# Gated linear attention with two expert layers: a new order of the first weights' product and unit 0, and three of its joins as plain fp32 matmuls

## Chip, cores and metric

One Trainium2 chip, one core. The metric is the device time of one execution in microseconds. TensorE (PE) does the matmuls and transposes, VectorE (DVE), ScalarE (ACT) and GpSimd (POOL) the elementwise work, and SyncE (SP) issues all DMAs, in one order.

## The reference

```python
for t in range(S):                        # q, k, v, f_logit: (4, 8, 768, 48)
    state = f[:, :, t, :, None] * state + einsum('bhd,bhe->bhde', k[:, :, t], v[:, :, t])
    y[:, :, t] = einsum('bhd,bhde->bhe', q[:, :, t], state)
x = y as (3072, 384)                      # f = sigmoid(f_logit)
h = x @ w_in                              # (384, 2048)
g = h if h >= 1, 0 if h <= -1, else (h + 1)**2 / 4
x = g @ w_out                             # (2048, 384)
out = ((x @ w1) * (x @ w2)) @ w3 @ w_last # (384, 1024) twice, (1024, 1024), (1024, 384)
```

All inputs are fp32. Since nothing stands between w3 and w_last (`moe2_w_out`), the kernel multiplies these two first and uses the product, w_joined (1024 x 384), in the last layer.

## The kernel before

**Units.** The 3072 tokens are 8 units of 384. For each unit there is an attention part and the first expert layer (w_in, gate, w_out), whose result goes to DRAM ("middle"). A second part then reads it in 6 groups of 512 and does the rest. Attention is done by halving blocks: within leaves of 4 tokens on VectorE and GpSimd (steps `gates`, `score0`, `sum`, `lag`, `prefix`, `query4`, `values`, `leaf_lag`, `leaf_add`), then transposes of the gates' total, of k and of q (`tot`, `k`, `q`), four levels of block scores (`level`, each followed on VectorE by masks, `k_next` and `q_next`, which the next level needs), key rows (`krow`), state updates (`update`), output (`y`) and its transposes (`x`).

**Precision.** Most matmuls run in three parts (`in_parts`, L1079): each operand is split in a high part, rounded to fp32r by ScalarE, and a low part, the difference, by VectorE; high by high, high by low and low by high are summed. The attention, the transposes and the fillers are plain fp32 matmuls.

**Joining w3 and w_last.** Eight row tiles of w3 are turned (`turn(t)`, L1085: 8 transposes into two banks), split by ScalarE (`turned_high`, L682) and VectorE (`turned_low`, L920) into two buffers, and joined with w_last (`join(t, part)`, L1098: 8 k tiles in 4 parts of 2, 24 matmuls in all). ScalarE copies the result (`joined_copy`, L689) and SyncE stores it to DRAM (L473). w_last itself is split once by `last_high` (L676) and `last_low` (L914); its low part takes the place of the raw values. All of this lies in the memory that w_out, x and g take later. So w_out is loaded after the joined rows have been stored (L474 to L478), and unit 0's `split_x` (L635) waits for that too.

**Order.** Each engine runs through the same positions, 32 to a unit; position 0 is where unit 0's first layer begins (`turn_of_units`: `up(0)`, `up(1)`). At odd positions TensorE does an `up` (w_in, 9 matmuls), at even ones a `down` (w_out, 9 matmuls). Tables written out by hand say at which position each step of the attention stands: `K_AT`, `LEVEL_AT` and the like (L236 to L243) for units 1 to 7, `UNIT0_AT` and `FIRST_AT` (less 32) for unit 0 and `NEXT_AT` for the steps ahead of unit 1. `JOIN_AT` (less 32) places the turns and the join parts, `LAST_AT` w_last's split, `PIECE_AT` the splits of w_in and w_out in 14 pieces. Within a position TensorE does attention first, then turns and joins, then `up` or `down`. Each engine executes strictly in its own order, so what stands behind a waiting instruction waits too. Narrow attention steps take one of three banks in turn, wide ones (`level`, `krow`, `update`, `y`) two of them; a step waits until the bank's last reader is done (`wait_bank`).

**Fillers.** `keep_running(n)` (L1151) issues n matmuls of the identity by itself whose result nobody reads: 40 before turn 0, 12 before turn 1, 12 before join 0, 9 before level 1 and 20 before level 3 of unit 0, 93 in all.

In TensorE's order, ahead of the first layer, the kernel has: turns 0, 1; total; join 0 among the transposes of k and q; turn 2, half of join 1; levels 0 to 3 with the rest of join 1 and turn 3; join 2 around the key rows; update 0; most of join 3; y 0; all other joins and turns at a stretch; then y 1, x 0, update 1, y 2, x 1, x 2, mixed with unit 1's first transposes.

Of the kernel before, what the change touches and what calls it, by code (L numbers as in the profile page):

```python
# [38 lines left out]
JOIN_PARTS = 4  # L39
GPSIMD_PIECES = ()  # L40
HEAD_ROWS = 64
GROUP = 512
BEFORE_TURN, BEFORE_JOIN, BEFORE_LEVEL = {0: 40, 1: 12}, 12, (0, 9, 0, 20)
# [51 lines left out]
def first_part(nc, given):  # L95
# [17 lines left out]
    with ExitStack() as ctx:  # L113
# [40 lines left out]
        pieces = halves_in[0:KD] + pairs_out[0:KD] + halves_in[KD:] + pairs_out[KD:]  # L154

        def in_piece(half, kk):
            return 2 * KD * half + kk

        def out_piece(i):
            return KD + i // 2 + (KD if i // 2 >= KD else 0)  # L160
# [4 lines left out]
              for n, o in (("hi", "w_out_hi"), ("lo", "w_out_lo"))]  # L165
        w3s = place("w3_rows", [P, 4, F2], over="x_hi")
# [5 lines left out]
        for name, shape in (("w1", [P, KD, F2]), ("w2", [P, KD, F2]), ("w_joined", [P, T2, DM])):  # L172
# [69 lines left out]
        GATES_AT, SCORE0_AT, SUM_AT, LAG_STEPS_AT, PREFIX_AT, QUERY_AT = 15, 1, (17, 27), (21, 22), 20, 28  # L242
        VALUES_AT, LEAF_LAG_AT, LEAF_ADD_AT = 17, 30, (31, 31)  # L243
# [158 lines left out]
        def _(sp):  # L402
# [89 lines left out]
            sp.wait_ge(joined_out, 16 * T2)  # L492
# [82 lines left out]
        def _(act):  # L575
# [161 lines left out]
        def _(dve):  # L737
# [176 lines left out]
            def last_low():  # L914
                for t in range(0, T2, 2):
# [4 lines left out]
            def turned_low(t):  # L920
                for half in range(2):
# [45 lines left out]
        def _(pe):  # L967
# [117 lines left out]
            def turn(t):  # L1085
# [306 lines left out]
```

## Time and profile before

| | |
|---|---|
| median of 3 runs | 948.19 us (947.43 to 951.37) |
| profiled execution | 946.54 us, of it 944.6 span |
| TensorE busy | 924.0 us, 98% |
| weight loads busy | 860.0 us, 91% |
| VectorE, ScalarE, GpSimd busy | 526.3, 392.5, 148.6 us |
| mean granted TensorE clock | 0.99 |
| chain that ended last | TensorE 93%, VectorE 5% |
| moved by DMA | 57.67 MB |

Idle time of an engine counts only where it lies on the chain that sets the end. Matmuls are pipelined: the duration of one (334 ns for 384 columns) is longer than the distance from one start to the next, and it is the distance that sets the pace. The trace names tiles by their place in memory: the w3 rows are `w_rows`, the turned ones `w_turned_hi` and `w_turned_lo`, the identity `ident`. A granted clock of 1.0 is 2.4 GHz, of 0.5 it is 1.2 GHz.

### The profile page before, as it was taken

Reading aid. Unit: us, or ns where it says so; the run is one execution under the profiler, and the core shown is the slowest. Engines: PE = TensorE matmul, PEld = TensorE weight load, DVE = VectorE, ACT = ScalarE, POOL = GpSimd, SP = SyncE. Lnnn points to the kernel's source line nnn. Section 1 sums busy time; section 2 is a strip of 40 time slices with the busy share of each in tenths; the row PEclk is TensorE's granted clock in tenths of the full one; section 3 lists DMA queues with packets and bytes.
Section 4 is the critical chain, followed back from the end, with each engine's and each line's share of the span. In section 5 each row is a group of like instructions: output and inputs, shape, how many; then the busy total and the mean of one; then the engine's idle time right before and its main releaser. Section 6 shows DMA issues by size and latency. Waiting matters only on the chain.

```text
span 944.6 us, 24359 instructions
## 1 busy us (share of the span) xinstructions
PE 924.0 (98%) x10722; PEld 860.0 (91%) x10722; DVE 526.3 (56%) x956; ACT 392.5 (42%) x766; POOL 148.6 (16%) x151
## 2 busy tenths in 40 slices
PE   6999799999999999999999999999999999999998
PEld 6989799999999999999999999998888888888887
DVE  6766698767767767768768664463222122213122
ACT  1433555645544644644644544674222222222212
POOL 2414104305205115115125000000000000000000
PEclk9999799999999999999999999999999999999999
DMA  9931820260340430530520200602020202000000
GB/s 267 247 119 43 210 52 2 66 88 2 78 76 2 89 66 2 97 58 1 112 43 2 52 2 2 248 12 93 1 67 1 67 1 68 1 34 0 34 1 34
DMA packets 115834, 57.67 MB, mean 61 GB/s; under 512 B 92433, under 2 KB 111121, under 8 KB 115217
## 3 DMA queue, kind: packets, MB, share of 16 engines
q1 hardware_dynamic: 115728, 56.11, 24.9%
q8 instruction: 85, 1.39, 0.6%
q14 instruction: 21, 0.16, 0.1%
HBM read 45.09 MB, written 11.01 MB: 59 GB/s over the span
## 4 chain that ended last, share of the span: by engine, by line
PE 93%; DVE 5%; DMA 1%; ACT 1%; issue 1%; SPq 0%; DVEq 0%; ACTq 0%
PE bank L1081 16%; PE bank L1083 15%; PE bank L1082 15%; PE bank L1327 11%; PE bank L1326 11%; PE bank L1325 10%; PE bank L1019 4%; PE bank L1056 2%; PE bank L1030 1%; PE bank L1062 1%; PE bank L1043 1%; PE bank L993 1%; DMA first_q<-in_q_dram 1%; PE bank L988 1%; PE bank L998 1%; PE bank L1076 1%
## 5 line engine op out<-in xcount | busy, mean ns | idle before, releaser
L1295 DVE TENSOR_TENSOR product<-bank,a_copy 128x512 f32<-128x512 f32 x48 | 33.2, 692 | 221.1 <-PE bank L1327 221.1
L1081 PE MATMUL bank<-x_hi,w_in_hi 128*128 128x384 f32 x384 | 135.4, 353 | 0.5 <-DVE x_lo L900 0.5
L1081 PE MATMUL bank<-g_hi,w_out_hi 128*128 128x384 f32 x384 | 133.6, 348 | 0.3 <-DVE g_lo L911 0.3
L1083 PE MATMUL bank<-x_hi,w_in_lo 128*128 128x384 f32 x384 | 129.2, 337 | 0.0
L1082 PE MATMUL bank<-x_lo,w_in_hi 128*128 128x384 f32 x384 | 129.0, 336 | 0.0
L1083 PE MATMUL bank<-g_hi,w_out_lo 128*128 128x384 f32 x384 | 128.7, 335 | 0.0
L1082 PE MATMUL bank<-g_lo,w_out_hi 128*128 128x384 f32 x384 | 128.6, 335 | 0.0
L657 ACT ACTIVATE g_hi<-gated 128x384 fp32r<-128x384 f32 x128 | 67.2, 525 | 128.2 <-DVE gated L906 128.2
L1327 PE MATMUL bank<-y_hi,w_lo 128*128 128x512 f32 x288 | 112.8, 392 | 0.0
L1326 PE MATMUL bank<-y_lo,w_hi 128*128 128x512 f32 x288 | 112.7, 391 | 0.0
L1325 PE MATMUL bank<-y_hi,w_hi 128*128 128x512 f32 x288 | 112.0, 389 | 0.0
L1249 ACT ACTIVATE a_copy<-bank 128x512 f32<-128x512 f32 x48 | 28.7, 598 | 187.2 <-PE bank L1327 187.2
L906 DVE SCALAR_TENSOR_TENSOR gated<-bank,gated 128x384 f32<-128x384 f32 x128 | 70.9, 554 | 59.6 <-ACT gated L651 59.5
L648 ACT ACTIVATE gated<-bank 128x384 f32<-128x384 f32 x128 | 62.4, 488 | 98.9 <-PE bank L1083 98.9
L911 DVE TENSOR_TENSOR g_lo<-gated,g_hi 128x384 fp32r<-128x384 f32 x128 | 71.6, 560 | 21.9 <-ACT g_hi L657 21.9
L1081 PEld LDWEIGHTS bank<-x_hi,w_in_hi 128*128 128x128 f32 x384 | 72.5, 189 | 2.8 <-DVE w_out_lo L392 0.6
L1081 PEld LDWEIGHTS bank<-g_hi,w_out_hi 128*128 128x128 f32 x384 | 72.0, 188 | 2.7 <-DVE g_lo L911 0.9
L534 POOL TENSOR_TENSOR y_leaf<-q_leaf,k_leaf 96x384 f32<-96x384 f32 x28 | 32.8, 1197 | 264.6 <-PE bank L998 234.9
L1082 PEld LDWEIGHTS bank<-x_lo,w_in_hi 128*128 128x128 f32 x384 | 72.6, 189 | 0.0
L1083 PEld LDWEIGHTS bank<-x_hi,w_in_lo 128*128 128x128 f32 x384 | 72.4, 188 | 0.0
L1082 PEld LDWEIGHTS bank<-g_lo,w_out_hi 128*128 128x128 f32 x384 | 72.2, 188 | 0.0
L1083 PEld LDWEIGHTS bank<-g_hi,w_out_lo 128*128 128x128 f32 x384 | 72.1, 188 | 0.0
(115 smaller groups left out, 1729.7 us busy)
## 6 DMA issues: line engine op xcount, KB each, us to landing
v_leaf<-in_v_dram SPq DMA_DIRECT2D x8, 576.0 KB, 6.5
v_rows<-in_v_dram SPq DMA_DIRECT2D x64, 72.0 KB, 2.7
middle<-middle_out SPq DMA_DIRECT2D x8, 576.0 KB, 3.3
w_rows<-in_moe_w_dram SPq DMA_DIRECT2D x8, 512.0 KB, 10.1
f_leaf<-in_f_logit_dram SPq DMA_DIRECT2D x28, 144.0 KB, 3.8
k_leaf<-in_k_dram SPq DMA_DIRECT2D x28, 144.0 KB, 4.6
q_leaf<-in_q_dram SPq DMA_DIRECT2D x28, 144.0 KB, 4.4
out_dram<-out_rows SPq DMA_DIRECT2D x5, 768.0 KB, 4.0
```

The lines of the kernel that those rows point to most:

```text
L648: nc.scalar.activation(gt[:, i % RING], h_bank[i % 2][:, 0:UNIT], ACT.Relu, bias=0.5, scale=0.5)\
L657: nc.scalar.activation(g[0][:, i % RING], gt[:, i % RING], ACT.Copy).then_inc(sems["g_hi"], 1)
L906: nc.vector.scalar_tensor_tensor(gt[:, i % RING], h_bank[i % 2][:, 0:UNIT], 1.0, gt[:, i % RING], ALU.max, ALU.min).then_inc(sems["gated"], 1)
L911: nc.vector.tensor_tensor(g[1][:, i % RING], gt[:, i % RING], g[0][:, i % RING].bitcast(F32), ALU.subtract)\
L1019: last = nc.tensor.matmul(wide[to:to + keys, pair // 2, o:o + HALF], kw[head_rows(ab), pair, at_:at_ + keys], later_half, start=True, stop ...
L1081: nc.tensor.matmul(o, w[0], b[0], start=first, stop=False)
L1082: nc.tensor.matmul(o, w[0], b[1], start=False, stop=False)
L1083: return nc.tensor.matmul(o, w[1], b[0], start=False, stop=last_)
L1295: nc.vector.tensor_tensor(pf[:, f % RING], b_bank[f % 2][:, 0:GROUP], af[:, f % 2], ALU.mult)\
L1325: nc.tensor.matmul(o, w[0], b[0], start=first, stop=False)
L1326: nc.tensor.matmul(o, w[0], b[1], start=False, stop=False)
L1327: return nc.tensor.matmul(o, w[1], b[0], start=False, stop=last_)
```

## The change

- Joins 0 to 2 (`PLAIN = 3`) are plain fp32 matmuls of the turned w3 rows by raw w_last, one per k tile. Their turned rows are copied by ScalarE unrounded and have no low part. The next turn waits for ScalarE's copy there, no longer for VectorE's low part.
- w_last comes in four loads, each with its own semaphore, behind the first w3 rows; part n of join 0 waits for load n. w_last's split stands behind update 0, its low part waits for join 2, and part n of join 3 waits for its share of it.
- The tables are new. TensorE's order ahead of the first layer becomes: turns 0, 1; total; join 0 among the transposes of k and q; level 0; turn 2, half of join 1, leaf 0, level 1, rest of join 1, leaf 1, level 2; turn 3, level 3, leaf 2; join 2 around the key rows, update 0; y 0, turn 4, join 3 with x 0, y 1, update 1, x 1, y 2 between its parts; turn 5, join 4 with x 2 before its last part; turn 6, join 5, turn 7, joins 6 and 7; then k 0, total, q 0, k 1, q 1, q 2 of unit 1. On VectorE the prefix of unit 0 comes behind the sums, w_last's low split ahead of y 0's add, and unit 1's lag steps on either side of turn 7's low part.
- Fillers: 20 before turn 0, 16 before turn 1, 3 before level 0, 8 before level 1, 8 before level 3, 55 in all.
- Of w_out's four loads only the last waits for the stored joined rows. Unit 0's `split_x` waits for turn 6, and its first `high` for the first four stored joined rows.
- All six pieces of w_in are split ahead of w_out's eight.

```diff
+PLAIN = 3
...
-BEFORE_TURN, BEFORE_JOIN, BEFORE_LEVEL = {0: 40, 1: 12}, 12, (0, 9, 0, 20)
+BEFORE_TURN, BEFORE_JOIN, BEFORE_LEVEL = {0: 20, 1: 16}, 0, (3, 8, 0, 8)
...
-        pieces = halves_in[0:KD] + pairs_out[0:KD] + halves_in[KD:] + pairs_out[KD:]
+        pieces = halves_in + pairs_out
...
+        wt_plain = place("w3_turned_plain", [P, 2, T2, P], over="w3_turned_hi")
...
-        K_AT, TOTAL_AT, Q_AT = (-7, -4, -1, 1), -3, (-2, -1, 0, 0)
-        Q_NEXT_AT, K_NEXT_AT = (3, 7, 9, 15), (4, 7, 11, 13)
-        LEVEL_AT = (3, 7, 9, 12)
-        LEAF_AT, KROW_AT, UPDATE_AT, Y_AT, X_AT = (8, 9, 15), (15, 22), (16, 25), (18, 23, 28), (23, 27, 29)
+        K_AT, TOTAL_AT, Q_AT = (-7, -1, 2, 2), -2, (-2, -1, -1, 0)
+        Q_NEXT_AT, K_NEXT_AT = (6, 7, 8, 14), (5, 7, 11, 12)
+        LEVEL_AT = (4, 7, 9, 12)
+        LEAF_AT, KROW_AT, UPDATE_AT, Y_AT, X_AT = (7, 11, 13), (15, 20), (16, 25), (18, 23, 28), (20, 28, 29)
...
-        LAST_AT, MASKS_AT = -43, -60
-        JOIN_AT = (-49, -47, -37, -37, -26, -25, -24, -18, -17, -13, -9, -9, 4, 7, 9, 12, 12, 13, 13, 14, 15, 15, 15, 15, 16, 16, 16, 16, 17, 18, 18, 18, 18, 18, 19, 19, 19, 20, 21, 21)
+        LAST_AT, MASKS_AT = 10, -60
+        JOIN_AT = (-47, -46, -44, -37, -34, -29, -24, -24, -16, -13, -13, -5, 1, 4, 10, 11, 12, 12, 13, 15, 16, 16, 17, 17, 17, 18, 18, 18, 18, 18, 19, 19, 20, 20, 21, 22, 22, 22, 22, 22)
...
-        PIECE_AT = (-8, 6, 18, 28, 29, 30, 31, 33, 33, 36, 39, 43, 43, 44)
-        FIRST_AT = (-56, -55, -58, -57, -57, -61, -60, -58, -44, -60, -40, -29, -24)
-        UNIT0_AT = (23, 28, 29, -33, -30, -27, -24, -41, -29, -29, -27, -25, -14, -14, -8, -1, -14, -11, -6, 6, 9, 13, 24, 15, 22, 26, -16, -17, -10, -13, -6, -9, 7, -3, 30)
-        NEXT_AT = (4, 28, 12, 19, 20, 15, 17, 14, 23, 27, 26, 32, 37)
+        PIECE_AT = (-7, 3, 4, 17, 20, 26, 28, 29, 31, 37, 37, 38, 41, 43)
+        FIRST_AT = (-55, -39, -60, -58, -55, -62, -62, -54, -50, -58, -41, -34, -27)
+        UNIT0_AT = (13, 15, 18, -36, -33, -27, -27, -45, -35, -35, -32, -27, -25, -14, -8, -4, -15, -9, -2, 3, 6, 10, 14, 12, 13, 16, -16, -20, -14, -12, -8, -10, 6, -4, 19)
+        NEXT_AT = (18, 27, -30, 18, 25, 18, 21, -17, 22, 30, 27, 34, 38)
...
+            def load_w_last(part):
+                src = w_last[F2 * part // JOIN_PARTS:F2 * (part + 1) // JOIN_PARTS, :].rearrange("(t p) n -> p t n", p=P)
+                sp.dma_start(wl_raw[:, T2 * part // JOIN_PARTS:T2 * (part + 1) // JOIN_PARTS], src).then_inc(w_last_in[part], 16)
+
             load_first()
-            sp.dma_start(wl_raw[:], w_last.rearrange("(t p) n -> p t n", p=P)).then_inc(w_last_in, 16)
-            for t in range(4):
+            load_w3(0)
+            for part in range(JOIN_PARTS):
+                load_w_last(part)
+            for t in range(1, 4):
                 load_w3(t)
...
-                sp.dma_start(w_joined[:, t], joined_rows(t)).then_inc(joined_out, 16)
-            sp.wait_ge(joined_out, 16 * T2)
+                sp.dma_start(w_joined[:, t], joined_rows(t)).then_inc(first_joined_out if t < T2 // 2 else joined_out, 16)
             for n in range(WO_LOADS):
+                if n == WO_LOADS - 1:
+                    sp.wait_ge(first_joined_out, 16 * (T2 // 2))
+                    sp.wait_ge(joined_out, 16 * (T2 // 2))
...
-                    act.wait_ge(joined_out, 16 * T2)
+                    act.wait_ge(turned, 2 * (T2 - 1))
...
+                elif i == 0:
+                    act.wait_ge(first_joined_out, 16 * (T2 // 2))
...
             def last_low():
+                dve.wait_ge(joined, PLAIN)
...
-                for half in range(2):
+                for half in range(2) if t >= PLAIN else ():
...
                 for kk in range(T2 * part // JOIN_PARTS, T2 * (part + 1) // JOIN_PARTS):
-                    last = in_parts(y_acc[t % 2][:, 0:DM], [w[:, t % 2, kk] for w in wt], [w[:, kk] for w in wl],
-                                    kk == 0, kk == T2 - 1)
+                    if t < PLAIN:
+                        last = nc.tensor.matmul(y_acc[t % 2][:, 0:DM], wt_plain[:, t % 2, kk], wl_raw[:, kk],
+                                                start=kk == 0, stop=kk == T2 - 1)
+                    else:
+                        last = in_parts(y_acc[t % 2][:, 0:DM], [w[:, t % 2, kk] for w in wt], [w[:, kk] for w in wl],
+                                        kk == 0, kk == T2 - 1)
```

## Rows read from the trace of the kernel before

**Rows 1.** Busy time by stage: length, PE, PEld, DVE, ACT, POOL; then clock, DMA share, GB/s.

```profile
0.00:92.45 92.45, 81.43 (x1086) 78.08 (x1089) 65.29 (x85) 29.13 (x49) 29.31 (x44) 0.98 0.64 171
92.45:108.19 15.74, 10.13 (x210) 8.20 (x210) 8.40 (x24) 6.01 (x13) 5.02 (x6) 0.64 0.79 236
108.19:944.60 836.41, 832.49 (x9431) 773.75 (x9431) 452.65 (x848) 357.32 (x706) 114.22 (x102) 1.00 0.20 46
```

**Rows 2.** Timeline of TensorE, 0 to 110: start, us, line, operands, count, [idle before].

```profile
2.85 11.66 PE L1154 MATMUL bank<-ident 128*128 128x128 f32 x80 [2.85 <-POOL ident L508]
...
17.41 2.84 PE L1154 MATMUL bank<-ident 128*128 128x128 f32 x24
24.03 1.16 PE L1094 MATMUL bank<-ident,w_rows 128*128 128x128 f32 x8 [3.77 <-DVE w_turned_lo L923]
25.03 0.76 PE L981 MATMUL bank<-ident,f_leaf 96*112 96x96 f32 x4
...
39.94 1.60 PE L1019 MATMUL bank<-q_cols,k_cols 48*64 48x32 f32 x96
...
44.74 1.60 PE L1019 MATMUL bank<-q_cols,k_cols 48*64 48x32 f32 x96 [0.99 <-DVE scores L860]
...
57.24 1.01 PE L1019 MATMUL bank<-q_cols,k_cols 48*32 48x32 f32 x96 [0.56 <-DVE q_cols L819]
...
60.41 1.11 PE L1030 MATMUL bank<-ident,k_cols 48*64 48x48 f32 x48 [0.88 <-DVE scores L860]
...
70.74 0.33 PE L1056 MATMUL bank<-v_rows,scores 64*64 64x48 f32 x8
```

**Rows 3.** Timeline of TensorE: 21 matmuls of a join, and the first layer's first.

```profile
79.44 0.33 PE L1081 MATMUL bank<-w_last_hi,w_turned_hi 128*128 128x384 f32 x1
...
82.91 0.34 PE L1083 MATMUL bank<-w_last_hi,w_turned_lo 128*128 128x384 f32 x1
...
108.19 0.66 PE L1081 MATMUL bank<-x_hi,w_in_hi 128*128 128x384 f32 x1 [0.28 <-DVE x_lo L900]
```

**Rows 4.** Timeline of VectorE, 0 to 130.

```profile
20.74 2.54 DVE L776 TENSOR_REDUCE leaf_scores<-score_lags 96x48 f32<-96x2304 f32 x1
...
28.33 4.18 DVE L918 TENSOR_TENSOR w_last_lo<-w_last_raw,w_last_hi 128x768 fp32r<-128x768 f32 x4
...
68.20 2.44 DVE L879 SCALAR_TENSOR_TENSOR state<-state,total_chunk,bank 112x48 f32<-112x48 f32 x12
```

**Rows 5.** Busy time by stage, 25.4 to 28.4: the granted clock is third from the end.

```profile
25.40:28.40 3.00, 3.00 (x16) 3.00 (x15) 3.00 (x4) 3.00 (x5) 3.00 (x3) 0.50 0.90 225
```

**Rows 6.** Timeline of GpSimd: one blocked multiply, then unit 1's prefix, queries and values.

```profile
26.75 4.95 POOL L554 TENSOR_TENSOR y_leaf<-v_leaf,leaf_scores 96x384 f32<-96x384 f32 x1
...
83.11 3.61 POOL L541 TENSOR_TENSOR f_leaf<-f_leaf 96x384 f32<-96x384 f32 x3 [13.72 <-DVE k_leaf L787]
86.89 4.76 POOL L548 TENSOR_TENSOR q_leaf<-q_leaf,f_leaf 96x384 f32<-96x384 f32 x4 [0.17 <-POOL f_leaf L541]
...
94.28 3.18 POOL L554 TENSOR_TENSOR y_leaf<-v_leaf,leaf_scores 96x384 f32<-96x384 f32 x4
```

**Rows 7.** The w_out load: its issue, the queue's wait, us to landing, ScalarE's first split.

```profile
94.87 2.26 SPq L478 DMA_DIRECT2D w_out_raw<-in_moe_w_out_dram  x4
...
SPq L478 <- DMA w_joined<-joined_rows: 1.5, 1, 1.5
...
w_out_raw<-in_moe_w_out_dram SPq DMA_DIRECT2D x1, 768.0 KB, 4.6
...
104.03 0.83 ACT L664 ACTIVATE w_out_hi<-w_out_raw 128x768 fp32r<-128x768 f32 x1
```

**Rows 8.** TensorE's longest wait from 120 to 660, and unit 2's levels 0 and 1.

```profile
PE bank L1019 <- DVE k_cols L838: 0.3, 1, 0.3
...
186.99 1.60 PE L1019 MATMUL bank<-q_cols,k_cols 48*64 48x32 f32 x96
...
194.97 1.60 PE L1019 MATMUL bank<-q_cols,k_cols 48*64 48x32 f32 x96
```

More of the change, by code:

```diff
@@ L153, in first_part @@
                      for t in range(0, T1, 2)]
-        pieces = halves_in[0:KD] + pairs_out[0:KD] + halves_in[KD:] + pairs_out[KD:]
+        pieces = halves_in + pairs_out
         def in_piece(half, kk):
-            return 2 * KD * half + kk
+            return KD * half + kk
         def out_piece(i):
-            return KD + i // 2 + (KD if i // 2 >= KD else 0)
+            return 2 * KD + i // 2
         wl = [place(f"w_last_{n}", [P, T2, DM], F32R, over=o) for n, o in (("hi", "w_out_hi"), ("lo", "w_out_lo"))]
@@ L201, in first_part @@
         w_landed = [ctx.enter_context(nc.semaphore(f"w_landed{i}")) for i in range(KD + WO_LOADS)]
-        w_last_in, wl_hi, wl_lo, turned, turned_hi, turned_lo, joined, joined_ev, y_first_in = (
+        wl_hi, wl_lo, turned, turned_hi, turned_lo, joined, joined_ev, y_first_in = (
             ctx.enter_context(nc.semaphore(n)) for n in (
-                "w_last_in", "w_last_hi", "w_last_lo", "turned", "turned_hi", "turned_lo", "joined", "joined_evacuated",
+                "w_last_hi", "w_last_lo", "turned", "turned_hi", "turned_lo", "joined", "joined_evacuated",
                 "y_first_in"))
-        joined_out = ctx.enter_context(nc.semaphore("joined_out"))
+        first_joined_out, joined_out = (ctx.enter_context(nc.semaphore(n)) for n in ("first_joined_out", "joined_out"))
+        w_last_in = [ctx.enter_context(nc.semaphore(f"w_last_in{i}")) for i in range(JOIN_PARTS)]
         given["first"].update(second)
@@ L234, in first_part @@
         ROUND = 2 * T1
[L236 to L239 removed]
+        K_AT, TOTAL_AT, Q_AT = (-7, -1, 2, 2), -2, (-2, -1, -1, 0)
+        Q_NEXT_AT, K_NEXT_AT = (6, 7, 8, 14), (5, 7, 11, 12)
+        LEVEL_AT = (4, 7, 9, 12)
+        LEAF_AT, KROW_AT, UPDATE_AT, Y_AT, X_AT = (7, 11, 13), (15, 20), (16, 25), (18, 23, 28), (20, 28, 29)
         SPLIT = 30
[L242 to L246 removed]
+        GATES_AT, SCORE0_AT, SUM_AT, LAG_STEPS_AT, PREFIX_AT, QUERY_AT = 16, 14, (17, 27), (21, 22), 24, 30
+        VALUES_AT, LEAF_LAG_AT, LEAF_ADD_AT = 17, 31, (31, 31)
+        LAST_AT, MASKS_AT = 10, -60
+        JOIN_AT = (-47, -46, -44, -37, -34, -29, -24, -24, -16, -13, -13, -5, 1, 4, 10, 11, 12, 12, 13, 15, 16, 16, 17, 17, 17, 18, 18, 18, 18, 18, 19, 19, 20, 20, 21, 22, 22, 22, 22, 22)
         MASK_JOIN_AT = -62
[L248 to L251 removed]
+        PIECE_AT = (-7, 3, 4, 17, 20, 26, 28, 29, 31, 37, 37, 38, 41, 43)
+        FIRST_AT = (-55, -39, -60, -58, -55, -62, -62, -54, -50, -58, -41, -34, -27)
+        UNIT0_AT = (13, 15, 18, -36, -33, -27, -27, -45, -35, -35, -32, -27, -25, -14, -8, -4, -15, -9, -2, 3, 6, 10, 14, 12, 13, 16, -16, -20, -14, -12, -8, -10, 6, -4, 19)
+        NEXT_AT = (18, 27, -30, 18, 25, 18, 21, -17, 22, 30, 27, 34, 38)
         steps = [(at, ("x", n)) for n, at in enumerate(X_AT)]
@@ L346, in turned_rows @@
         def turned_rows(part, t, half):
-            return wt[part][:, t % 2, half * T2 // 2:(half + 1) * T2 // 2].rearrange("p k n -> p (k n)")
+            to = wt_plain if t < PLAIN else wt[part]
+            return to[:, t % 2, half * T2 // 2:(half + 1) * T2 // 2].rearrange("p k n -> p (k n)")
         def padded_pair(t, pair, j):
@@ L491, in _ @@
                 sp.dma_start(second[name][2][:], src.rearrange("(k p) n -> p k n", p=P)).then_inc(later_in[n], 16)
-            sp.wait_ge(joined_out, 16 * T2)
+            sp.wait_ge(joined_out, 16 * (T2 // 2))
             sp.dma_start(second["w_joined"][2][:], w_joined).then_inc(later_in[2], 16)
@@ L676, in last_high @@
             def last_high():
-                act.wait_ge(w_last_in, 16)
                 for t in range(0, T2, 2):
+                    act.wait_ge(w_last_in[t * JOIN_PARTS // T2], 16)
                     hi, raw_ = (w[:, t:t + 2, :].rearrange(flat) for w in (wl[0], wl_raw))
@@ L1089, in turn @@
                 for half in range(2):
-                    if t:
-                        pe.wait_ge(turned_lo, 2 * (t - 1) + half + 1)
+                    if t > PLAIN:
+                        pe.wait_ge(turned_lo, 2 * (t - 1 - PLAIN) + half + 1)
+                    elif t:
+                        pe.wait_ge(turned_hi, 2 * (t - 1) + half + 1)
                     for j in range(T2 // 2):
@@ L1102, in join @@
                         keep_running(BEFORE_JOIN)
+                    pe.wait_ge(w_last_in[part], 16)
+                if t == PLAIN:
                     pe.wait_ge(wl_lo, T2 // 2 * (part + 1) // JOIN_PARTS)
                 if part == 0:
-                    pe.wait_ge(turned_lo, 2 * t + 2)
+                    if t < PLAIN:
+                        pe.wait_ge(turned_hi, 2 * t + 2)
+                    else:
+                        pe.wait_ge(turned_lo, 2 * (t - PLAIN) + 2)
                     if t >= 2:
@@ L1108, in join @@
                 for kk in range(T2 * part // JOIN_PARTS, T2 * (part + 1) // JOIN_PARTS):
-                    last = in_parts(y_acc[t % 2][:, 0:DM], [w[:, t % 2, kk] for w in wt], [w[:, kk] for w in wl],
-                                    kk == 0, kk == T2 - 1)
+                    if t < PLAIN:
+                        last = nc.tensor.matmul(y_acc[t % 2][:, 0:DM], wt_plain[:, t % 2, kk], wl_raw[:, kk],
+                                                start=kk == 0, stop=kk == T2 - 1)
+                    else:
+                        last = in_parts(y_acc[t % 2][:, 0:DM], [w[:, t % 2, kk] for w in wt], [w[:, kk] for w in wl],
+                                        kk == 0, kk == T2 - 1)
                 if part == JOIN_PARTS - 1:
@@ L1116, in up @@
                     wait(pe, "gated", u, i - 1)
+                elif u == 0:
+                    pe.wait_ge(turned_lo, 2 * (T2 - 1 - PLAIN) + i + 1)
                 if u == 0 and i % (T1 // 2) == 0:
```

## Prediction

> **Where the time goes now.** I read the stages first [rows 1]. From 108.19 us, where the first matmul of the first layer starts, to the end TensorE is busy for 832.5 of 836.4 us at full clock, and the change adds or removes no matmul there. The page's first part says the same of the whole: TensorE 98% busy, VectorE 56%, ScalarE 42%, GpSimd 16%. What it can win lies in the 108.2 us ahead: in the first 92.45 us w3 and w_last are joined beside unit 0's attention, in the next 15.7 us unit 0's tail runs alone, TensorE 10.1 us busy with a mean granted clock of 0.64.
>
> Next TensorE in order of time [rows 2]. The first two rows shown are fillers (`keep_running`); a filler is two instructions of some 0.11 us each (24 in 2.84 us). The kernel has 93 fillers, 80 of their 186 instructions in 11.66 us at the start. The reader is to see the marks of the attention chain: total transposed at 25.03, level 0 at 39.94, level 1 at 44.74, level 3 at 57.24, the keys' rows at 60.41, first y at 70.74. Three of them idle behind VectorE, so VectorE's steps between levels set the pace. Joins fill the holes: 21 matmuls in 3.47 us plus one step, 0.1735 us each [rows 3], 4.17 us a join (24 matmuls), 1.04 a part.
>
> **Plain joins.** Joins 0 to 2 lose the split: per k tile one fp32 matmul for three fp32r ones. Nothing here shows a plain one of 384 columns. A filler is plain, of 128 columns, and two instructions of 0.11; three times the columns give at most 0.33 an instruction, 0.66 a tile. The low bound is two instructions at the fp32r pace, 0.35; the high one four, 0.69. I take 0.66, nearest in kind: 1.32 a part, 5.28 a join, 1.11 more than now, +3.3 us for three (-4.2 to +4.0). It frees VectorE of three turned lows (3.8 us, estimated from 0.65 a half) and moves 4.18 us of w_last lows [rows 4] from 28.33 to behind join 2.
>
> **Start to level 0.** The first w3 rows and w_last are ahead of need in either order: join 0 now stands behind the total's transpose, and that waits for the prefix. VectorE does score, prefix and two sums, ending at 23.28 [rows 4]; the new order puts prefix last, so the total moves from 25.03 to 23.3. From there (durations without a row of their own are read off TensorE's timeline of the first 110 us, as start to start): transposes 0.6, four parts 5.3, eight groups of k and q at 0.4, three fillers 0.7: 9.8, level 0 at 33.1. But TensorE now has idled since turn 1 (over by about 19, when w3's second rows land). Before, an idle of 3.77 us [rows 2] was followed by 3.0 us at granted 0.50, that is 1.2 GHz [rows 5]. I take half clock from 23.3 to about 28.5: 2.6 us lost (0 to 2.6; which of the two hangs on how long the new gap of 4.3 us is in truth). Level 0 at 35.7, 4.2 earlier. Unit 0's `query4` (1.9 in VectorE's timeline) follows to 25.1, and the leaves' lag and adds, held by GpSimd, end near 35: in time for level 0's masks at 37.3. Should GpSimd end at 35.7, as it does now, they end at 38.7; level 1 still starts when TensorE is free. The Trainium skill, "TensorE: Matmul & The Clock Gate", section "Why this matters for your kernels", asks for continuous matmuls, since idle gaps throw the clock back; it speaks against the 38 fewer fillers, and the trace agrees by that row. By a rule that an idle gap is free the sum would be 2.6 us lower.
>
> **Levels.** Level 0 takes 1.6; behind it stand turn 2 (0.95), two parts, a leaf (0.35), eight fillers (1.8): level 1 at 43.0. From level 0 to 1 was 4.8 with 3.2 of VectorE work in it; now that is hidden. Level 1 1.6, two parts and a leaf: level 2 at 47.6, where VectorE also arrives. Level 2 1.6 and 3.0 of VectorE: level 3 at 52.2. Its 1.0, a w_in low (1.2), turn 3's low (1.3), masks and keys 2.1: key rows at 56.8 (before 60.41). Then the state update waits for ScalarE, which splits two w_in pieces (1.05 each in its timeline) between the two key-row copies: update at 61.2, rest of join 2 to 64.6. VectorE finishes 12 state steps (2.44) [rows 4] at 65.35, which frees the banks: first y at 65.4, 5.3 ahead of 70.74. But by 70.74 the old kernel also had turn 4 and three parts done, 4.1 us.
>
> **Rest of the joins.** Left are three y (1.0 each), three x (0.45), an update 0.75, four turns at 0.95, five joins 20.8: 29.8 us. Two waits are new. w_last's lows (4.18) stand on VectorE ahead of y 0's add, and x 0 waits for it: 1.5 us. y 2 waits for the second 12 state steps: 1.1. The last join ends at 65.4 + 29.8 + 2.6 = 97.8, against 92.45, with the tail inside it.
>
> **From last join to first layer.** Two chains run side by side. (a) The w_out load no longer waits for all joined rows: it was issued at 94.87, 1.5 us of that a wait [rows 7]; now 0.9 us after the join. It lands after 4.6, at 103.3; ScalarE then splits two pieces (0.83 each) ahead of unit 1's total and q 0: 105.7, and q 1, q 2 need those banks. (b) Unit 1's lag products now stand on VectorE behind the turn lows and end about 95.2; GpSimd's prefix 3.6 and query 4.8 [rows 6] follow: q 0 at 103.6. Both end together: first layer at 106.7, 1.5 us before 108.19. Half clock follows the idle as before, 2.2 us then; I take 1 us more of it, 0.5 lost.
>
> **The other units.** Level 0 moves one place later and level 1 stays. They start 8.0 us apart, now 6.3: 1.6 of level, three expert steps of 1.56. VectorE's work in those 4.7 us, by its own timeline from 188.73 on, is masks 1.0, keys 1.2, queries 0.9 and two gate steps 1.0, together 4.1; margin 0.6, so zero. Were the margin gone, each tenth would cost 0.7 us over seven units (0 to +2). Keys and queries of pairs 2 and 3, total, lag and update steps move by a place or two the same way, TensorE's and GpSimd's order of them being kept but for q 1 and q 2 ahead of the turn; I cost them at nothing, since TensorE finds its next work ready throughout. TensorE's longest wait there now is 0.3 [rows 8].
>
> **Sum.** 944.6 - 1.5 + 0.5 = 943.6 of span; with the 1.9 outside it this execution would take 945.5. Its own time, 946.5, lies 1.6 below the median of the runs, 948.2; from the median the sum is 947.2. I give 946.4, between.
>
> **Rivals.** *The clock holds* (or turn 1 comes later than I think): no half clock at 23.3, 2.6 us, and full clock from 106.7, 1.6 us: together 4.2 below the forecast, 942. For: a late w3 row leaves a shorter gap. Against: the gap of 4.3 us is longer than the one that cost the clock. *GpSimd blocked*, the slower one: chain (b) is now last, with VectorE's sum, w_in low and lag beside it. One of GpSimd's multiplies took 4.95 us while VectorE worked without a break, against 0.8 usually (four in 3.18) [rows 6]; each such block is 4.1 more. One is +2.6 net; two of the seven put the first layer at 114.9 and the time at 946.4 + 8.2, 954.6. It decides once chain (b) is over 6.5 us late. Against: in the same work now (3.61 and 4.76) none was seen. The Trainium skill, "SBUF — State Buffer", section "Who interferes with whom", says one of the two engines blocks fully while the other holds the shared port; the 4.95 agrees. *It doesn't do what it says*: w3 first and w_last in four loads win nothing, since the prefix is last; that is in my forecast, and if a plain tile costs 0.35 the joins win 2 us more, still within noise: 944.5.
>
> **Chances.** A measurement of this kernel tells 0.5% from no change: 4.7 us. Forecast 0.58 (0.05 of it faster), the clock holds 0.22, GpSimd blocked 0.10, cheap plain joins 0.10. Faster 0.27, same 0.63, slower 0.10. The range reaches into the clock case, 941.0, and to one block, 951.0.
>
> **What would show it.** Plain records of about 0.33 us spacing, 48; a granted 0.5 around 23 to 28; total at 23.3, level 0 near 35.7, first y near 65; an idle ahead of x 0 ended by VectorE; last join near 98; first layer near 106.7 released by the q copies; then 836 us as before. Wrong if the first layer starts before 103 or after 111, or if that last stretch differs by over 2 us.

## The result and the profile after

The changed kernel takes 952.75 us in the median of 20 runs (946.76 to 956.0), the kernel before 947.14 on the same chips (20 runs): a ratio of 1.0057, 95% interval 1.0045 to 1.0068, so slower by 0.57%. That is past the 0.5% that the prediction calls no change, though the interval begins just below it, and the time lies outside its range of 941.0 to 951.0. The profiled execution took 952.83, of it 950.9 span; that span is 6.3 more than before. First the stages, cut at the same two events as in [rows 1]: end of the last join part, first matmul of the first layer.

```profile
0.00:101.30 101.30, 83.62 (x1170) 71.08 (x1171) 69.67 (x103) 33.19 (x56) 20.86 (x39) 0.93 0.58 156
101.30:110.76 9.46, 3.33 (x25) 3.00 (x23) 7.05 (x5) 5.06 (x9) 9.29 (x7) 0.76 0.84 288
110.76:950.90 840.14, 834.00 (x9433) 774.36 (x9431) 458.36 (x844) 353.93 (x702) 120.69 (x107) 1.00 0.21 47
```

The last join ends 8.85 us later than before, the tail behind it is 6.28 shorter, and from the first layer on it takes 3.73 more. The prediction had +5.35, -6.8 and +0.5. In the last stage 1.5 us of the 3.7 are busy time (834.0 against 832.5), the rest is idle time, 6.1 us in place of 3.9. The granted clock of the first stage fell from 0.98 to 0.93.

TensorE's timeline of the changed kernel, the marks of [rows 2] and the new waits:

```profile
23.06 0.89 PE L996 MATMUL bank<-ident,f_leaf 96*112 96x96 f32 x4 [4.51 <-DVE f_leaf L776]
...
34.71 1.60 PE L1034 MATMUL bank<-q_cols,k_cols 48*64 48x32 f32 x96 [0.24 <-ACT q_cols L610]
...
54.26 0.26 PE L1034 MATMUL bank<-q_cols,k_cols 48*32 48x32 f32 x5 [1.77 <-issue]
...
57.39 1.37 PE L1045 MATMUL bank<-ident,k_cols 48*64 48x48 f32 x48
...
66.14 0.33 PE L1071 MATMUL bank<-v_rows,scores 64*64 64x48 f32 x8 [0.59 <-DVE state L893]
...
71.50 0.52 PE L1091 MATMUL bank<-ident,y_rows 128*128 128x128 f32 x3 [2.11 <-DVE y_rows L901]
...
79.26 0.33 PE L1071 MATMUL bank<-v_rows,scores 64*64 64x48 f32 x8 [1.13 <-DVE state L893]
...
108.27 0.86 PE L1008 MATMUL bank<-ident,q_leaf 96*112 96x96 f32 x4 [5.65 <-POOL q_leaf L560]
...
110.76 0.67 PE L1096 MATMUL bank<-x_hi,w_in_hi 128*128 128x384 f32 x1
...
128.92 1.84 PE L1034 MATMUL bank<-q_cols,k_cols 48*64 48x32 f32 x96 [1.49 <-DVE q_cols L833]
...
143.08 1.01 PE L1034 MATMUL bank<-q_cols,k_cols 48*32 48x32 f32 x96 [0.59 <-DVE k_cols L852]
...
152.76 0.76 PE L1058 MATMUL bank<-v_rows,k_rows 64*48 64x48 f32 x48 [0.79 <-ACT k_rows L625]
```

The reader is to see five waits of 1.5 us and over, from the total on: ahead of the total, inside level 3 (an "issue": TensorE stood still and the profile shows nothing that it waited for; 91 of the level's 96 matmuls were done; I call this the instruction wait), ahead of x 0, ahead of unit 1's q 0, and ahead of its level 1. The next view is busy time by stretch of the same kernel, with the granted clock third from the end. Behind or in each of the five lies one at about half clock:

```profile
21.20:28.00 6.80, 4.94 (x11) 2.99 (x12) 5.99 (x6) 0.90 (x2) 4.95 (x3) 0.52 1.20 239
55.30:58.70 3.40, 3.40 (x53) 1.92 (x51) 1.25 (x3) 0.22 (x1) 0.00 (x0) 0.54 0.05 17
72.35:75.75 3.40, 3.40 (x65) 3.14 (x58) 1.08 (x4) 0.49 (x1) 0.00 (x0) 0.54 0.02 5
106.50:113.30 6.80, 5.03 (x25) 5.06 (x26) 4.84 (x4) 4.65 (x8) 6.80 (x5) 0.52 1.10 357
130.40:133.80 3.40, 3.40 (x28) 3.33 (x23) 3.40 (x7) 0.90 (x2) 0.00 (x0) 0.54 0.01 4
```

In three of them TensorE is busy throughout, so that up to half their length, 1.7 us each, is lost; the kernel before had its long stretch of half clock in the tail, where TensorE mostly had nothing to do ([rows 1], clock 0.64). The Trainium skill, "TensorE: Matmul & The Clock Gate", section "Why this matters for your kernels", warns of idle gaps, and the length that it gives for them is longer than any of these three; the waits of 1.8, 2.1 and 1.5 us here were followed by half clock as well, so for this kernel the measurement decides: shorter ones can count too.

Two waits have their cause on the other engines, in the timelines of VectorE (w_last's lows, then unit 0's round) and GpSimd (unit 1's prefix and queries):

```profile
65.95 5.07 DVE L933 TENSOR_TENSOR w_last_lo<-w_last_raw,w_last_hi 128x768 fp32r<-128x768 f32 x4
...
125.50 1.83 DVE L396 TENSOR_TENSOR w_out_lo<-w_out_raw,w_out_hi 128x768 fp32r<-128x768 f32 x2 [0.20 <-ACT w_out_hi L678]
...
127.72 0.95 DVE L833 TENSOR_TENSOR q_cols<-q_cols,total 112x768 f32<-112x768 f32 x1
```

```profile
63.86 4.61 POOL L546 TENSOR_TENSOR y_leaf<-q_leaf,k_leaf 96x384 f32<-96x384 f32 x4 [32.77 <-DVE q_cols L833]
...
98.38 3.59 POOL L553 TENSOR_TENSOR f_leaf<-f_leaf 96x384 f32<-96x384 f32 x3 [29.91 <-DVE k_leaf L801]
102.13 5.99 POOL L560 TENSOR_TENSOR q_leaf<-q_leaf,f_leaf 96x384 f32<-96x384 f32 x4 [0.17 <-POOL f_leaf L553]
```

The lows took 5.07 us in place of 4.18 [rows 4], and GpSimd's four multiplies, 63.86 to 68.47, lie beside their first half. The chain of work that ended last in the changed kernel (start, length, what) parts them:

```profile
66.04 3.03 DVE w_last_lo L933 x2
69.21 1.81 DVE w_last_lo L933 x2
```

Two beside GpSimd took 1.5 us each, two without it 0.9. `query4` took 5.99 in place of 4.76 [rows 6]. And level 1 of unit 1 waits for queries that stand on VectorE behind two w_out lows.

### The profile page after: what moved, and what is told of

Same layout as the page of the kernel before. It is cut to its first block, busy times and chain, and to the rows that moved or that the text cites. A ratio compares the mean times of both kernels' runs of the same rounds, so it can differ in the third digit from the quotient of the medians.

```text
span 950.9 us, 24157 instructions
## 1 busy us (share of the span) xinstructions
PE 920.9 (97%) x10622; PEld 848.4 (89%) x10622; DVE 535.1 (56%) x950; ACT 392.2 (41%) x766; POOL 150.8 (16%) x151
## 4 chain that ended last, share of the span: by engine, by line
PE 90%; DVE 5%; issue 1%; DMA 1%; POOL 1%; ACT 1%; SPq 0%; DVEq 0%; POOLq 0%
PE bank L1096 15%; PE bank L1098 14%; PE bank L1097 14%; PE bank L1355 10%; PE bank L1354 10%; PE bank L1353 10%; PE bank L1034 5%; PE bank L1132 2%; PE bank L1071 2%; PE bank L1045 1%; PE bank L1008 1%; PE bank L1077 1%; PE bank L1003 1%; PE bank L1058 1%; DMA first_q<-in_q_dram 1%
## 5 line engine op out<-in xcount | busy, mean ns | idle before, releaser
L925 DVE TENSOR_TENSOR g_lo<-gated,g_hi 128x384 fp32r<-128x384 f32 x128 | 75.9, 593 | 32.0 <-ACT g_hi L671 32.0
L546 POOL TENSOR_TENSOR y_leaf<-q_leaf,k_leaf 96x384 f32<-96x384 f32 x28 | 35.0, 1277 | 239.5 <-PE bank L1013 206.7
```

Of the source, the lines that this page charges most:

```text
L546: nc.gpsimd.tensor_tensor(yl[:, j], qj[:, j], kj[:, j], ALU.mult)\
L925: nc.vector.tensor_tensor(g[1][:, i % RING], gt[:, i % RING], g[0][:, i % RING].bitcast(F32), ALU.subtract)\
```

## The experiments

Each was timed against the kernel before on its own chip, where that took 946.6 to 946.7. "After" is the changed kernel, 952.75.

| run | what it is | median us | ratio (95%) |
|---|---|---|---|
| f1_fill | after, 48 more fillers | 946.62 | 0.9996 (0.9987 to 1.0005) |
| f2_pieces | after, last w_out splits later | 952.6 | 1.0057 (1.0042 to 1.0073) |
| f3_plain0 | after, no plain joins | 957.04 | 1.0105 (1.0092 to 1.0118) |
| f4_addfirst | after, w_last's split behind y 0's add | 953.45 | 1.006 (1.0046 to 1.0073) |
| g1_steady | f1, old tables for units 1 to 7 | 943.32 | 0.9963 (0.9951 to 0.9975) |
| g2_pieces | f1, last w_out splits later | 944.98 | 0.9986 (0.9978 to 0.9995) |
| g3_bfill | before, fillers at start and tail | 946.41 | 0.9989 (0.998 to 0.9999) |
| g4_all | g1, fewer fillers, two orders mended | 940.53 | 0.9945 (0.9929 to 0.9962) |
| h1_fillplain0 | f1, no plain joins | 959.04 | 1.013 (1.0115 to 1.0146) |
| h2_tailfill | before, fillers in the tail alone | 945.09 | 0.9983 (0.9973 to 0.9994) |
| h3_nofill | g4 without its added fillers | 947.45 | 1.0005 (0.9995 to 1.0015) |
| h4_lastfirst | f1, w_last loaded ahead of w3 | 952.22 | 1.0052 (1.0037 to 1.0066) |

**Is it the clock?** Fillers in three of the waits, and nothing else.

```diff
+BEFORE = {(0, "tot"): 18, (0, "x", 0): 8, (1, "q", 0): 22}
...
                     keep_running(BEFORE_LEVEL[n])
+                keep_running(BEFORE.get((u, *grp), 0))
```

> The changed kernel with fillers in three of its idle gaps, none longer than the gap: 18 ahead of unit 0's total (gap 4.5 us), 8 ahead of x 0 (2.1 us), 22 ahead of unit 1's q 0 (5.6 us). Theory clock (the gaps let the clock fall, and half clock after them is what costs): the granted clock rises from 0.987 to about 0.993, the half clock after 23, after 72 and after 106 is gone, and the time falls by 1.5 to 2 us for each of the three, 4 to 6 us in all, to about 947. Theory waits (the gaps themselves cost, the clock is a symptom): the fillers change the clock and not the time, 952 to 953. Theory plain price: no change either.

946.62, 6.1 less than the changed kernel (5.8 by the two ratios), with more for TensorE to do. Its timeline:

```profile
22.94 0.54 PE L998 MATMUL bank<-ident,f_leaf 96*112 96x96 f32 x4 [0.45 <-DVE f_leaf L777]
...
32.31 1.60 PE L1036 MATMUL bank<-q_cols,k_cols 48*64 48x32 f32 x96 [0.23 <-ACT q_cols L611]
...
49.12 1.01 PE L1036 MATMUL bank<-q_cols,k_cols 48*32 48x32 f32 x96 [0.38 <-DVE q_cols L834]
...
61.52 0.33 PE L1073 MATMUL bank<-v_rows,scores 64*64 64x48 f32 x8 [0.60 <-DVE state L894]
...
96.51 5.10 PE L1184 MATMUL bank<-ident 128*128 128x128 f32 x44
102.36 0.51 PE L1010 MATMUL bank<-ident,q_leaf 96*112 96x96 f32 x4 [0.75 <-POOL q_leaf L561]
...
104.16 0.42 PE L1098 MATMUL bank<-x_hi,w_in_hi 128*128 128x384 f32 x1
```

The total starts when it did (22.94), but level 0 is 2.4 us earlier, first y 4.6 and the first layer 6.6. Level 3 runs in one piece of 96: the instruction wait is gone too. So the fillers did more than their theory says. Of the 6.6 us, 2.4 come between the total and level 0, where nothing but the clock differs; 1.4 between the first y and the last join, and 0.6 behind it. The other 2.2 come between level 3 and the first y, where this run adds no filler: the instruction wait and the half clock behind it went together, and the run doesn't part them. Without these 2.2 the theory's places give 4.4. Its stretches, with the clock third from the end, show full clock from the total to the first layer; the wait of 1.49 us ahead of unit 1's level 1 has no filler, and half clock follows it:

```profile
22.90:104.16 81.26, 74.68 (x1164) 64.31 (x1164) 59.37 (x91) 32.76 (x59) 23.89 (x19) 1.00 0.52 146
122.80:129.60 6.80, 6.80 (x65) 6.74 (x58) 4.61 (x8) 2.03 (x4) 0.00 (x0) 0.50 0.23 49
```

**The wait in unit 0's round.** The last five w_out splits moved from positions 37 to 43 to 42 to 58, behind unit 1's queries, on the changed kernel and on f1.

```diff
-        PIECE_AT = (-7, 3, 4, 17, 20, 26, 28, 29, 31, 37, 37, 38, 41, 43)
+        PIECE_AT = (-7, 3, 4, 17, 20, 26, 28, 29, 31, 42, 46, 50, 54, 58)
```

> The changed kernel with the last five w_out splits placed shortly ahead of their use (positions 10, 14, 18, 22, 26 of unit 0 for 5, 5, 6, 9, 11). If the 3.7 us that came after the first layer's start are VectorE's burst of w_out lows ahead of unit 1's level 1 (idle 1.5 + 0.6 + 0.8 us and 3.4 us at half clock behind it), the stretch from the first layer to the end falls from 840.1 to about 836.4 and the time by 3.5 to 4 us, to 949. If they come from the new places of the levels and key rows in units 1 to 7, the stretch stays near 840.

952.6, nothing won: the wait of 1.49 is gone, but three of about 1 us stand later in the round (1.05 for k, 1.03 for the key rows, 1.08 ahead of an x), and the instruction wait in level 3 was 2.4 us in this run. A wait moved, not removed.

> The filled kernel with the last five w_out splits later (positions 10, 14, 18, 22, 26). In the run without fillers this took away the wait ahead of level 1 and put two of 1.0 us behind level 2 and the key rows. Here the clock is full when the first layer starts, so what these waits do to the clock shows: 839 us after the first layer's start and 944.5 if they do not lower it, 841 and 946.5 if they do.

944.98, 1.6 less than f1: the same waits of about 1 us, and behind them no half clock, so that from the first layer on it takes 838.5 us instead of f1's 841.1. On the changed kernel, too, that stage went from 840.1 to 839.2, but the first layer was 0.5 later.

**The plain joins.** The changed kernel, and then f1, with all joins split; `LAST_AT` as in the kernel before, since join 0 then needs both parts of w_last.

```diff
-PLAIN = 3
+PLAIN = 0
...
-        LAST_AT, MASKS_AT = 10, -60
+        LAST_AT, MASKS_AT = -43, -60
```

> The changed kernel with no plain joins: all eight in three parts, w_last split at its old place ahead of join 0. Theory plain price (0.66 us a tile, 1.1 us more for each join on TensorE, and w_last's lows in a worse place): 3 to 5 us faster, 948 to 950. Theory clock: join 0 waits for the split from 25 to about 30, level 0 comes near 40 again, so the last join ends no earlier; within 2 us of 952.7 either way.

957.04, 4.3 us slower instead of faster.

> The changed kernel with the fillers of the first experiment (18 ahead of unit 0's total, 8 ahead of x 0, 22 ahead of unit 1's q 0) and joins 0 to 2 in three parts again, w_last split ahead of join 0 as in the kernel before. With plain joins these fillers gave 946.6. Theory (the plain joins are worth something only because w_last's split and turn 0's low part then stand on VectorE ahead of turn 1 and join 0, so turn 1 waits some 9 us and everything behind it is late): about 950.5, 4 us more than with plain joins, as without the fillers (957.0 against 952.7). Rival (what the plain joins saved there was granted clock, which the fillers give back): 947 or less, as 3.3 us of TensorE work go away (1.1 a join).

959.04: 12.4 slower than f1, three times what the theory asked. TensorE's timeline of f3 (first row) and of h1 (the other fence):

```profile
26.21 1.94 PE L1111 MATMUL bank<-ident,w_rows 128*128 128x128 f32 x8 [9.03 <-DVE w_turned_lo L938]
```

```profile
26.14 1.94 PE L1113 MATMUL bank<-ident,w_rows 128*128 128x128 f32 x8 [7.88 <-DVE w_turned_lo L939]
...
33.10 0.50 PE L998 MATMUL bank<-ident,f_leaf 96*112 96x96 f32 x4
```

Turn 1 waits for turn 0's low part, which starts on VectorE at 25.4, behind all leaf steps up to `query4`; with plain joins turn 1 starts at about 17.4, with fillers and without. In h1 the 18 fillers then follow it (5.4 us here, partly at half clock, where they took 4.2 in f1 and filled a wait), and the total comes at 33.10 in place of 22.94. Behind that h1 also has two instruction waits, 2.42 us ahead of join 0 and 2.09 in level 2, though it has all of f1's fillers; how much of its 12.4 us they make wasn't parted. So a plain join does cost TensorE what the prediction said, and what it wins here is that VectorE's splits leave the start. The theory named the right wait; that fillers placed for one order become plain cost in the other it did not foresee. I read 4.3 us as what it costs to take the plain joins out of this order. It is no fair price of them by themselves: the tables were made for plain joins, and the kernel before, whose tables put turn 0's low part ahead of `query4`, has 3.77 us at the same place where f3 waits 9.03 [rows 2]. An order of split joins with new tables of its own was not run.

**Load order.** f1 with all of w_last ahead of w3's first rows.

```diff
-            load_w3(0)
             for part in range(JOIN_PARTS):
                 load_w_last(part)
-            for t in range(1, 4):
+            for t in range(4):
                 load_w3(t)
```

> The changed kernel with the fillers of the first experiment and w_last's four loads issued ahead of w3's first rows, otherwise the same; it stood at 946.6 with w3's rows first. Theory (turn 0 stands behind the first fillers and its rows land ahead of need only when first): turn 0 starts later by the time that 1.5 MB take, and as VectorE's first steps cover the total's wait, what is lost is hidden behind the fillers ahead of the total: 946.1 to 947.1. Rival (turn 0 and turn 1 and so the whole start shift by some 4 us): 950.

952.22: the rival is right. TensorE's timeline:

```profile
16.74 1.97 PE L1112 MATMUL bank<-ident,w_rows 128*128 128x128 f32 x8 [7.82 <-DMA w_rows<-in_moe_w_dram]
...
24.11 1.04 PE L1112 MATMUL bank<-ident,w_rows 128*128 128x128 f32 x8
...
29.00 0.49 PE L997 MATMUL bank<-ident,f_leaf 96*112 96x96 f32 x4
```

Turn 0 starts at 16.74 instead of 11.89, the fillers behind it run at half clock, and the total, ready on VectorE since about 23, starts 6.1 us later.

**w_last's lows behind y 0's add.** `LAST_AT` 12 for 10, on the changed kernel.

> The changed kernel with w_last's split behind y 0's add on VectorE and ScalarE instead of ahead of it. The idle of 2.1 us ahead of x 0 is gone, join 3's first part waits about 1 us more. Theory clock: the half clock after 72 goes with it, 1.0 + 1.7 us, so 2 to 3 us faster, 950. Theory waits: 1 us faster, 951.7.

953.45, unchanged within the scatter. The wait ahead of x 0 is gone, one of 1.4 us ahead of join 3 (for the same lows) has come, and the first layer starts 2.7 us earlier in the profile; but that execution (950.65) lies at the low end of its runs (950.35 to 954.09), and the median doesn't show the gain. In that execution the instruction wait was 0.96 us, and no half clock follows it or stands around 72. Nothing follows but that the wait ahead of x 0 can be exchanged for another.

**The tables of units 1 to 7.** f1 with the kernel before's.

```diff
-        K_AT, TOTAL_AT, Q_AT = (-7, -1, 2, 2), -2, (-2, -1, -1, 0)
-        Q_NEXT_AT, K_NEXT_AT = (6, 7, 8, 14), (5, 7, 11, 12)
-        LEVEL_AT = (4, 7, 9, 12)
+        K_AT, TOTAL_AT, Q_AT = (-7, -4, -1, 1), -3, (-2, -1, 0, 0)
+        Q_NEXT_AT, K_NEXT_AT = (3, 7, 9, 15), (4, 7, 11, 13)
+        LEVEL_AT = (3, 7, 9, 12)
...
-        GATES_AT, SCORE0_AT, SUM_AT, LAG_STEPS_AT, PREFIX_AT, QUERY_AT = 16, 14, (17, 27), (21, 22), 24, 30
+        GATES_AT, SCORE0_AT, SUM_AT, LAG_STEPS_AT, PREFIX_AT, QUERY_AT = 15, 1, (17, 27), (21, 22), 20, 28
```

> The filled kernel (946.6), with the tables for units 1 to 7 of the kernel before and all else new. In the filled kernel 841.2 us follow the first layer's start, 836.4 in the kernel before; behind it lie waits of 1.5, 0.6 and 0.8 us in unit 0's round and 6.8 us at half clock. Theory tables (levels, keys and queries packed one place closer leave no room for the w_out lows): with the old tables this stretch falls to 837 to 838, the time to 943. Theory w_out burst alone: the splits at positions 5, 5, 6 still stand ahead of the queries, the stretch stays at 840 to 841 and the time at 946.

943.32, 3.3 less than f1. From the first layer on it is 838.5 us; one wait is left in unit 0's round, 1.8 us for k. So the new tables cost about 2.6 us there (841.1 less 838.5), and by the waits they lie in unit 0's round: from one level 3 to the next, units 2 to 7 take 69.2 us each with either set of tables. The theory of the tables has it: 838.5 is half a microsecond above its 837 to 838, and the time is its 943.

**Does the old order gain from fillers as much?** First at its start and in its tail, then in the tail alone.

```diff
+BEFORE = {(0, "update", 1): 6, (0, "y", 2): 9, (1, "k", 1): 5}
...
-BEFORE_TURN, BEFORE_JOIN, BEFORE_LEVEL = {0: 40, 1: 12}, 12, (0, 9, 0, 20)
+BEFORE_TURN, BEFORE_JOIN, BEFORE_LEVEL = {0: 40, 1: 28}, 12, (0, 9, 0, 20)
```

> The kernel before, with fillers in its own gaps: 16 more ahead of turn 1 (3.8 us), 6 ahead of update 1 (1.4), 9 ahead of y 2 (2.2), 5 ahead of unit 1's k 1 (1.1). Theory clock: its 17 us at half clock, over TensorE work of some 8 us in the tail and 3 us after 25.4, cost about 4 us, so 942.5 to 943.5, and the new order with fillers (946.6) is then slower than the old one by its own waits in unit 0's round. If the old order does not gain, the clock costs only where the new order puts matmuls behind short waits, and fillers leave it at 946.5.

946.41 in the median, 0.2 less: missed. Level 0 came 1.8 us later (41.75): turn 1 started 0.9 later behind its 28 fillers (24.97 for 24.03), and `query4` took 3.04 us on VectorE for 1.88. But the median hides two groups. Five of the 12 runs took 943.6 to 944.9 us, and the two at a mean clock of 1.0 took 943.62 and 944.02; the other seven, the profiled one among them, took 946.1 to 947.3. So with full clock the old order too gains some 3 us, most of what the theory asked. Hence the second, with that number at 12 again:

> The kernel before with fillers in its tail alone (6 ahead of update 1, 9 ahead of y 2, 5 ahead of unit 1's k 1), its start as it was. Before, the clock is at half for 13.7 us from the last join on, TensorE busy 10.1 of 15.7 us there. Theory (the old tail's end is set by VectorE and ScalarE, whose steps fillers don't shorten; the clock costs at most the 1.3 us or so of matmuls after the last wait): 945.5 to 946.6, first layer at 107.0 or later. Rival (the half clock costs the tail 3 us or more, as it cost the new order 6): 943.5 or less, first layer near 105.

945.09, 1.6 less than before and between the two: just below the theory's 945.5 to 946.6, with the first layer at 106.16 instead of 108.19, where the theory said 107.0 or later and the rival 105:

```profile
106.16 0.66 PE L1083 MATMUL bank<-x_hi,w_in_hi 128*128 128x384 f32 x1 [0.80 <-DVE x_lo L901]
```

The half clock did not go away here, it moved: in this execution it lies from 104.9 to 111.7, ahead of and in the first layer, and another 3.4 us of it follow the wait of 2.47 ahead of turn 0. So 1.6 us is what these fillers win, and no measure of what all the half clock cost the old order; g3's two runs at full clock say about 3. The new order's 24 us of it, with the instruction wait, were worth about 6.

**Together.** g1 with 10 instead of 22 fillers ahead of q 0, unit 1's first lag step two positions earlier, and the w_out splits spread.

```diff
-        NEXT_AT = (18, 27, -30, 18, 25, 18, 21, -17, 22, 30, 27, 34, 38)
+        NEXT_AT = (18, 27, -30, 18, 25, 18, 19, -17, 22, 30, 27, 34, 38)
...
-        PIECE_AT = (-7, 3, 4, 17, 20, 26, 28, 29, 31, 37, 37, 38, 41, 43)
+        PIECE_AT = (-7, 3, 4, 17, 20, 26, 32, 33, 35, 36, 39, 43, 43, 44)
```

> What the readings point to, together: the new order up to the last join with fillers ahead of the total, x 0 and q 0 (10 now), the old tables for units 1 to 7, unit 1's second lag step ahead of turn 7's low on VectorE, the first three w_out splits behind the first gate instead of ahead of unit 1's total, the others at the old places. The first layer starts near 101 (104.2 with fillers alone), 836.5 to 838 follow: span 938 to 939, time 940 to 941. If the lag step ahead of turn 7's low holds up join 7 instead, the first layer stays at 104 and the time at 943.

940.53, as forecast, and the fastest, 0.55% below the kernel before (ratio 0.9945, 0.9929 to 0.9962; four of the six runs took 940.2 to 940.5, two 943.9 and 945.0); the first layer starts at 100.65. And the same without the 36 fillers:

> The fastest version so far (940.5) without its 36 added fillers: the tables of the kernel before for units 1 to 7, unit 1's lag two steps earlier, w_in and w_out split in another order, and nothing else against the changed kernel. Theory (every short wait of TensorE of 1.5 us and over is followed by 3.4 us at half clock, 6 to 7 us lost in all, whatever the rest of the order): 946.5 to 948, with three or more half clock periods ahead of the first layer. Rival (the other edits took away the waits themselves, so that the fillers are worth little on this order): 942 or less.

947.45, 6.9 more (5.7 by the ratios): the theory's number, and from the first layer on both take 837.9 us, so all of it lies ahead. The instruction wait of 2.03 is in it and was not in the theory. Its timeline has the instruction wait and the wait ahead of x 0 back, and the stretches behind them are again at half clock:

```profile
54.58 0.32 PE L1034 MATMUL bank<-q_cols,k_cols 48*32 48x32 f32 x5 [2.03 <-issue]
...
71.78 0.88 PE L1091 MATMUL bank<-ident,y_rows 128*128 128x128 f32 x3 [2.11 <-DVE y_rows L901]
```

```profile
54.30:57.70 3.40, 3.12 (x13) 1.94 (x13) 1.98 (x4) 0.49 (x1) 0.00 (x0) 0.53 0.12 45
71.40:78.20 6.80, 6.42 (x123) 5.50 (x124) 2.47 (x8) 0.49 (x1) 0.00 (x0) 0.51 0.01 2
```

## Why the prediction was wrong

The time is 952.75 and not 946.4, and "slower" had a chance of 0.10; against the trace the sum was 945.5 and the execution 952.83, 7.3 us more. Of these 3.5 lie ahead of the last join's end (101.3 for 97.8), 0.6 between it and the first layer (9.46 for 8.9), 3.2 behind (840.1 for 836.9).

**Right.** The total at 23.06 (23.3) and the half clock behind it (21.2 to 28.0 for 23.3 to 28.5); a plain instruction at 0.33 us, 0.66 a tile; levels 0, 1 and 2 within 1.0 us (34.71, 41.99, 46.73); the first y (66.14 for 65.4), y 2's wait (1.13 for 1.1), an idle ahead of x 0 ended by VectorE; the w_out load no longer last in the chain: ScalarE had its first piece at 107.09, it ended at 108.6, and the queries' copies came after GpSimd. Units 2 to 7 unchanged. Two terms of the working don't add up as they are written: the key rows come to 57.8 and not 56.8 (57.39 in the trace), and chain (a) to 105.0 and not 105.7; neither makes the miss.

**Step 1 that failed: the clock was priced by two places.** The sum has 2.6 us behind the total and 0.5 at the first layer, and gives "two waits are new" their own length alone, 1.5 and 1.1. The trace has three more stretches of 3.4 us with TensorE busy at half clock, up to 1.7 lost in each, two of them ahead of the last join. f1 takes the fillers' way out and wins 6.1, 2.2 of it at the instruction wait of step 4; g4 and h3, the same order with and without, differ by 6.9. The rival *The clock holds* was the right mechanism with the wrong sign: the clock was the unknown, and it held less often than in my forecast, not more. I weighed the 38 fillers that the change took out for one gap and not for the others; whether they would have helped at their old places was not run.

**Step 2: "the other units" at zero.** I asked for the margin of VectorE in the steady units and found 0.6 us. That was right for units 2 to 7. In unit 0's round the w_out splits share VectorE with those steps; nothing in the sum looked there. There stand waits of 1.49, 0.59 and 0.79 and one stretch at half clock, and the stage took 3.7 us more than before, 3.2 more than in the sum; g1 shows that the tables for units 1 to 7 alone make 2.6 of f1's time there.

**Step 3: durations beside another engine.** w_last's lows at 4.18 were 5.07, `query4` at 4.76 was 5.99. The first two lows ran beside GpSimd's multiplies, and VectorE was busy for 7.05 of the 9.46 us around `query4`. The lows made the wait ahead of x 0 2.11 for 1.5. Of the 4.7 us by which q 0 was late (108.27 for 103.6), `query4` is 1.2; the rest is that unit 1's lag products ended at 98.3 for 95.2, with everything ahead of them late. The Trainium skill, "SBUF — State Buffer", section "Who interferes with whom", has one of the two wait while the other holds their port; the 1.5 us of a low beside GpSimd, for 0.9 without it, agree in kind. No run tested this apart. The rival *GpSimd blocked* priced a block at 4.1 us; 1.2 is what showed, so it didn't decide; that its 954.6 lies nearest to the measured time is chance.

**Step 4: the instruction wait.** 1.8 us in level 3 stand in no row of before. It was 1.8, 2.4, 1.0 and 2.0 us in after, f2, f4 and h3, and absent in f1, g1, g2, g4 and h4, which have more fillers ahead of it. But fillers are no sure remedy: h1 has them and two such waits. What holds TensorE there isn't shown, and whether the fillers help by their time or by their place in the program was not tried.

**The rival *It doesn't do what it says*.** The load order was written off ("ahead of need in either order", "win nothing"). h4 refutes that for the filled order: w_last first costs 5.6 us, as turn 0 then waits 7.82 us for its rows. My total at 23.3 rested on turn 1 being over by about 19, and that holds only with w3's first rows ahead. How much it is worth without the added fillers was not run.

And why was the change not faster? With full clock up to the first layer (f1) it only draws level, 946.6. The tail inside the joins (6.3) is paid for by a last join 8.9 later and by 3.7 in unit 0's round, and the plain joins (4.3 in this order) are already in these numbers. Old tables there and fillers in the waits make of the same idea a kernel 6.0 us faster than before by the medians, 5.2 by the ratio.

## What to carry to other kernels

When TensorE sets the time, price a new wait of 1.5 us and over not by its length alone but by the granted clock in the stretch behind it, for each wait, and fill those that can't be removed; and take the fillers out again where the wait is gone, since in another order (h1, and the start of g3) they are cost. A precision split taken away can be worth more by what it frees on the engine that made it than its matmuls cost. Check new tables in the unit where one-time work shares the engines, not only in the steady ones.

## What the runs showed of the hardware

- Over the changed kernel's 20 runs the time goes with the mean granted clock of the run: 946.8 us at 0.994, 950.0 to 951.7 at 0.989 to 0.991, 952.7 to 953.3 at 0.985 to 0.987, 953.9 to 956.0 at 0.982 to 0.984. It is one program throughout; only the execution of 952.83 was traced, so how its waits and its half clock vary from run to run isn't shown.
- The length of a wait alone doesn't tell whether the clock falls: behind 1.49 us it did for 3.4 us (after) and for 6.8 (f1), behind 1.62 us in g4 and 1.66 in h3, both for a w_out low, it didn't; ahead of turn 0 it didn't behind 2.31 us (after) and 2.47 (f1), but did behind 2.47 (h2), 2.65 (h1) and 3.12 (g1); behind 1.0 to 1.1 us (g2) it never did.
- A plain fp32 matmul of 384 columns is two instructions of 0.33 us each at full clock (eight in 2.77 us in f1), against three of 0.1735 for the split one [rows 3].
- TensorE stood still for 1.0 to 2.9 us (after, f2, f3, f4, h1, h3) where the profile shows no engine and no DMA that it waited for. The cause isn't known.
